# Gate on expert rows at the PSUM exit, hidden activations turned in halves, block sums behind the gathers: one change to a fused attention, expert and dense kernel

## The chip, the cores and the metric

One core of a Trainium2 chip. The metric is the device time of one launch, in microseconds (us). Engines: TensorE (PE; its weight loads are PEld), VectorE (DVE), ScalarE (ACT), GpSimd (POOL), SyncE (SP, which only issues DMAs); an engine's queue takes its instructions in order.

## The reference

```python
state = gamma*state + k[t] outer v[t];  y[t] = scale * q[t] @ state   # 4 batches, 8 heads, 768 steps, 64 wide
x = rows of y                                    # 3072 tokens x 512
logits = x @ w_gate + modality_bias[modality_id] # 8 experts
e = argmax(logits);  gate = softmax(logits)[e]
x = gate * (relu(x @ w1[e]) @ w2[e])             # w1 512x1024, w2 1024x512
h = x @ w_in;  out = (h * sigmoid(1.702*h)) @ w_out   # 2048 wide
```

## The kernel before

**Order of the work.** Attention over 24 tiles of 128 tokens writes x to HBM (x_rows). DVE works out the routing: tokens are sorted by expert into slots, each expert's slots padded to whole tiles of 128. With these inputs three experts get tokens, 13, 12 and 1 tiles, so used_tiles is 26 (the 26 stores of y_slots agree). Then the expert tiles run, and then the dense part in three groups of 1024 tokens: eight pairs of column blocks up (seven products each, P1, P5, P6, P3, P7, P2, P4), and the way down. All products are in three passes (hi*hi, hi*lo, lo*hi: L1519, L1520, L1521); a value's hi part is a copy by ACT, its lo part a subtraction by DVE.

**An expert tile i** (expert_step). PE: up(i), 24 multiplications; turn_rows, which turns the gathered x of tile i+1; down(i-1), 24 multiplications into ps_y, which needs both halves of hT_lo of tile i-1 and all of w2; turn_hidden(i), eight transposes (L1566). ACT: relu of the two halves of up(i) (L809), xT_hi(i+1), hT_hi(i) in two halves, and the issue of the stores of y(i-1). DVE: xT_lo(i+1) (L1146), take_y(i-1) (a copy of the slots' token numbers, L1229, and the copy of ps_y to y_out, L1230), then hT_lo(i) in two halves (L1206). The first 15 tiles are stored twice, to y_head and to y_slots.

**POOL's queue**, in order. gather_slots for tiles 0 to 4 (five buffers xg): a copy of indices (L569) and an indirect DMA (L571). pool_step(0): the gather of tile 5 and, where an expert begins (T_SPLIT), the split of the next expert's weights, eight pieces: a casting DMA (L589) and a subtraction (L578) each. Then two load_quads (L666), two mix_quads (four block sums, L673 to L678, and a store to w_comb, L681), and three rounds of: two load_quads, then five pool_step(k), with a mix_quads behind the second and third. pool_step(k) waits for gT_done of tile k, gathers tile k+5, and may split weights. After tile 15 come fetch_first (rows of y_head for the first group by L625, for each tile of tokens a gather of gates by L632, and the scaling by the gate, L639), more pool_steps, and for the later groups fetch: rows by L625, gates by L632; there ACT scales the rows (scale_rows, L872) behind pairs 2 and 5. At the end POOL scatters the output by indirect DMA (store_half, L688) and waits for out_stored.

**The loop over tiles that may not exist.** ACT and DVE run i from 24 to 30 with a test i < used_tiles, so that empty turns come behind the last tile.

## Time and profile before

| | us |
|---|---|
| median of 3 runs | 1022.33 |
| lowest, highest | 1018.75, 1022.68 |
| the profiled execution, its own time | 1028.59 |
| its span | 1027.0 |
| PE busy in the span | 967.7 |

The span runs from the first record to the last of one profiled execution; that execution has a time of its own beside the three runs. Busy time is the sum of an engine's instructions. The granted clock is a share of full speed.

### The profile page before, as it was taken

Reading aid. Unit: us, or ns where it says so; the run is one execution under the profiler, and the core shown is the slowest. Engines: PE = TensorE matmul, PEld = TensorE weight load, DVE = VectorE, ACT = ScalarE, POOL = GpSimd, SP = SyncE. Lnnn points to the kernel's source line nnn. Section 1 sums busy time; section 2 is a strip of 40 time slices with the busy share of each in tenths; the row PEclk is TensorE's granted clock in tenths of the full one; section 3 lists DMA queues with packets and bytes.
Section 4 is the critical chain, followed back from the end, with each engine's and each line's share of the span. In section 5 each row is a group of like instructions: output and inputs, shape, how many; then the busy total and the mean of one; then the engine's idle time right before and its main releaser. Section 6 shows DMA issues by size and latency. Waiting matters only on the chain.

```text
span 1027.0 us, 16695 instructions
## 1 busy us (share of the span) xinstructions
PE 967.7 (94%) x5947; PEld 786.6 (77%) x5948; DVE 470.5 (46%) x706; ACT 416.3 (41%) x672; POOL 254.1 (25%) x287
## 2 busy tenths in 40 slices
PE   7999789959999989999899999999999999999995
PEld 5778557848888868888678788877788888888884
DVE  2444384212222212214656586446668545665541
ACT  2333323212222212222666664446666445564441
POOL 4444143665124772200033001051200101000101
PEclk8999989979999999999999999999999999999998
DMA  8778357776236542100344124363313535222431
GB/s 277 242 248 240 113 208 261 231 254 216 107 130 223 182 137 72 50 25 25 120 145 125 57 86 144 104 224 106 121 51 94 144 118 183 90 82 83 142 103 42
DMA packets 50968, 143.86 MB, mean 140 GB/s; under 512 B 6092, under 2 KB 6260, under 8 KB 46788
## 3 DMA queue, kind: packets, MB, share of 16 engines
q1 hardware_dynamic: 29904, 84.97, 25.9%
q0 software_dynamic: 11440, 40.74, 11.8%
q10 hardware_dynamic: 9540, 17.10, 4.7%
q8 instruction: 45, 0.74, 0.3%
q14 instruction: 39, 0.32, 0.1%
HBM read 100.81 MB, written 33.59 MB: 131 GB/s over the span
## 4 chain that ended last, share of the span: by engine, by line
PE 83%; DMA 5%; issue 4%; ACT 3%; DVE 3%; POOL 2%; SPq 0%; POOLq 0%; ACTq 0%; DVEq 0%
PE bank L1519 23%; PE bank L1521 23%; PE bank L1520 23%; DMA raw<-w 2%; PE bank L1398 2%; PE bank L1424 2%; PE bank L1566 2%; PE bank L1433 1%; PE bank L1414 1%; PE bank L1385 1%; PE bank L1601 1%; PE bank L1528 1%; POOL weights L578 1%; PE bank L1444 1%; DMA qk_in<-qk 1%
## 5 line engine op out<-in xcount | busy, mean ns | idle before, releaser
L1521 PE MATMUL bank<-w_hi,act_lo 128*128 128x512 f32 x384 | 150.3, 391 | 0.0
L1519 PE MATMUL bank<-w_hi,act_hi 128*128 128x512 f32 x384 | 150.1, 391 | 0.0
L1520 PE MATMUL bank<-comb_lo,act_hi 128*128 128x512 f32 x384 | 150.0, 391 | 0.0
L1519 PE MATMUL bank<-mix_hi,w_hi 128*128 128x512 f32 x336 | 133.7, 398 | 10.0 <-ACT h_sum L738 8.0
L1521 PE MATMUL bank<-mix_hi,comb_lo 128*128 128x512 f32 x336 | 133.0, 396 | 0.0
L1520 PE MATMUL bank<-mix_lo,w_hi 128*128 128x512 f32 x336 | 132.1, 393 | 0.0
L738 ACT ACTIVATE w_hi<-comb 128x1024 fp32r<-128x1024 f32 x96 | 96.0, 1002 | 81.0 <-PE bank L1521 75.6
L688 POOL DMA_INDIRECT out<-f_out,token_idx x24 | 25.6, 1067 | 389.9 <-ACT f_out L738 383.0
L1282 DVE TENSOR_TENSOR comb_lo<-comb,w_hi 128x1024 fp32r<-128x1024 f32 x48 | 58.8, 1224 | 72.6 <-ACT w_hi L738 71.8
L1519 PE MATMUL bank<-weights,hT_hi 128*128 x208 | 85.9, 413 | 5.5 <-issue 4.0
L1288 DVE TENSOR_TENSOR h_sum<-bank,h_sum 128x512 f32<-128x512 f32 x72 | 49.5, 689 | 84.1 <-PE bank L1521 78.6
L1146 DVE TENSOR_TENSOR xT_lo<-bank,xT_hi 128x512 fp32r<-128x512 f32 x27 | 18.7, 692 | 146.8 <-ACT xT_hi L738 144.8
L1519 PE MATMUL bank<-weights,xT_hi 128*128 x208 | 83.1, 400 | 1.6 <-DVE xT_lo L1146 1.6
L1519 PEld LDWEIGHTS bank<-mix_hi,w_hi 128*128 128x128 f32 x336 | 63.7, 190 | 27.0 <-ACT h_sum L738 10.1
L1520 PEld LDWEIGHTS bank<-comb_lo,act_hi 128*128 128x128 f32 x384 | 72.1, 188 | 15.9
L1521 PEld LDWEIGHTS bank<-w_hi,act_lo 128*128 128x128 f32 x384 | 72.1, 188 | 15.7
L1519 PEld LDWEIGHTS bank<-w_hi,act_hi 128*128 128x128 f32 x384 | 72.1, 188 | 15.7
L1520 PE MATMUL bank<-weights,hT_hi 128*128 x208 | 83.0, 399 | 1.0 <-issue 1.0
L1521 PE MATMUL bank<-weights,hT_lo 128*128 x208 | 83.5, 401 | 0.4 <-issue 0.3
L738 ACT ACTIVATE hT_hi<-bank 128x512 fp32r<-128x512 f32 x52 | 28.3, 595 | 132.2 <-PE bank L1566 126.3
L1521 PE MATMUL bank<-weights,xT_lo 128*128 x208 | 81.5, 392 | 0.0
L1520 PE MATMUL bank<-weights,xT_hi 128*128 x208 | 81.3, 391 | 0.0
(178 smaller groups left out, 1636.9 us busy)
## 6 DMA issues: line engine op xcount, KB each, us to landing
comb<-w_comb SPq DMA_DIRECT2D x24, 1024.0 KB
comb<-w_out SPq DMA_DIRECT2D x48, 512.0 KB
qk_in<-qk SPq DMA_DIRECT2D x24, 512.0 KB, 3.7
raw<-w SPq DMA_DIRECT2D x24, 512.0 KB, 5.9
weights<-raw POOLq DMA_DIRECT2D x16, 512.0 KB, 4.6
w_comb<-mix_in POOLq DMA_DIRECT2D x8, 1024.0 KB, 4.2
y_slots<-y_out ACTq DMA_DIRECT2D x26, 256.5 KB
v_in<-v SPq DMA_DIRECT2D x24, 256.0 KB, 4.5
```

What stands on the lines that cost most here:

```text
L578: nc.gpsimd.tensor_tensor(lo, raw[:, i % RAW_BUFS, :], hi.bitcast(F32), ALU.subtract).then_inc(w_ready, 1)
L688: pool.indirect_dma_start(out=out, out_offset=bass.IndirectOffsetOnAxis(ap=token_idx[:, g % 2, j:j + 1], axis=0), in_=f_out[:, j, :], in_o ...
L738: copy = lambda dst, src: nc.scalar.activation(dst, src, ACT.Copy)
L1146: tt(xT_lo[:, :, :], ps_gT, xT_hi[:, :, :].bitcast(F32), ALU.subtract).then_inc(gT_split, 1)
L1282: tt(comb_lo[piece % COMB_BUFS][:, 0:PIECE], comb_f[piece % COMB_BUFS][:, 0:PIECE], w_hi[piece % HI_BUFS][:, 0:PIECE].bitcast(F32), ALU.su ...
L1288: tt(h_sum[:, at_, :], bank[k % 2][:, :], h_sum[:, at_, :], ALU.add).then_inc(h_ready, 1)
L1398: last = mm(ps_scores[par][keys, p, :], kT[rows, t % 2, p, keys], turned[rows, p, :], start=True, stop=True)
L1424: last = mm(x_place(h), v_in[:, t % IN_BUFS, h, :], masked[:, t % 2, (h % 2) * PAIRS + h // 2, :], start=(t % CHUNKS == 0 and h < 4), stop ...
L1519: mm(dst, hi, w_hi, start=first, stop=False, skip_group_check=skip)
L1520: mm(dst, hi, w_lo, start=False, stop=False, skip_group_check=skip)
L1521: return mm(dst, lo, w_hi, start=False, stop=last, skip_group_check=skip)
L1566: last = turn(ps_hT[s][:, a, :], hid[:, s * 4 + a, :], identity)
```

## The change

Gates by slot: POOL gathers the five first tiles' gates right behind gather_slots(0 to 4), and in pool_step(k), k > 0, that of tile k+4, after y_copied has reached k+1. take_y multiplies ps_y by the gate where it copied, and the scaling by POOL and ACT and the gathers of gates by token row are gone. y_copied now starts at 1, by a small copy of DVE ahead of its tile loop, behind which DVE waits for the five first gates. ACT turns gateT and stores gate_rows earlier.

Halves: down(i-1) and turn_hidden(i) are cut in two and alternate. DVE takes y behind hT_lo, and down waits for y_copied. The last tile's down goes into bank 6, and its take_y and store move into the first pair of the first group.

Block sums: the two first mix_quads and the two first load_quads of each round move behind pool_steps. The rest: a Sigmoid of one column behind hidden_hi(0); the empty turns of the tile loop come first on ACT and DVE; a pool.drain() ahead of the last group's stores, and the wait for out_stored moved from POOL to SP.

The core of the diff (declarations, the two fetch functions' calls of keep_index and the empty lines are left out):

```diff
@@ -204,7 +206,8 @@
         token_idx = keep("token_idx", [P, 2, GT], I32)
-        row_gate = keep("row_gate", [P, GT], F32)
+        sig_warm = keep("sig_warm", [P, 1], F32)
+        gate_slot = keep("gate_slot", [P, XG_BUFS], F32)
@@ -512,6 +516,7 @@
                     load_piece(g, k)
+            sp.wait_ge(out_stored, DMA_INC * GT * GROUPS)
@@ -572,6 +577,11 @@
                     xg_in[buf], DMA_INC)
+            def gather_gate(buf, tokens):
+                pool.indirect_dma_start(out=gate_slot[:, buf:buf + 1], out_offset=None, in_=gate_rows,
+                                        in_offset=bass.IndirectOffsetOnAxis(ap=tokens, axis=0)).then_inc(gate_in, DMA_INC)
@@ -591,11 +601,17 @@
                         take_lo(i, place(i), n_cast)
-            def pool_step(k, buf):
+            def pool_step(k, buf, first=False):
...
                     gather_slots(k + XG_BUFS, buf)
+                    if not first:
+                        hold(gate_in, DMA_INC * k + DMA_INC * (XG_BUFS - 1))
+                        hold(y_copied, k + 1)
+                        earlier = (buf - 1) % XG_BUFS
+                        gather_gate(earlier, slot_idx[:, earlier:earlier + 1])
@@ -615,9 +631,12 @@
                 gather_slots(k, k)
+            hold(gate_stored, DMA_INC)
+            for buf in range(XG_BUFS):
+                gather_gate(buf, token_of_slot[:, buf:buf + 1])
...
             used_tiles = steering(pool, T_TILES, TILES, MAX_TILES)
-            pool_step(0, 0)
+            pool_step(0, 0, True)
@@ -626,18 +645,10 @@
                                         ).then_inc(yg_in[j], DMA_INC)
-            def gather_gate(g, j, rows):
-                hold(yg_in[j], DMA_INC * g + DMA_INC)
-                pool.indirect_dma_start(out=row_gate[:, j:j + 1], out_offset=None, in_=gate_rows,
-                                        in_offset=bass.IndirectOffsetOnAxis(ap=rows[:, DM:ROW].bitcast(I32), axis=0)
-                                        ).then_inc(row_gate_in[j], DMA_INC)
+            def keep_index(g, j, rows):
+                pool.wait_ge(yg_in[j], DMA_INC * g + DMA_INC)
                 nc.gpsimd.tensor_copy(token_idx[:, g % 2, j:j + 1], rows[:, DM:ROW].bitcast(I32)).then_inc(token_idx_ready, 1)
-            def scale_first(j, rows):
-                pool.wait_ge(row_gate_in[j], DMA_INC)
-                nc.gpsimd.tensor_tensor(rows[:, 0:DM], rows[:, 0:DM],
-                                        row_gate[:, j:j + 1].to_broadcast([P, DM]), ALU.mult).then_inc(yg_scaled, 1)
@@ -689,20 +698,20 @@
                         in_=f_out[:, j, :], in_offset=None).then_inc(out_stored, DMA_INC)
-            hold(gate_stored, DMA_INC)
...
                 load_quads(buf, buf)
-            for buf in range(MIX_BUFS):
-                mix_quads(buf, buf, 1)
             with pool.Fori(0, HEAD_LOOPS) as it:
-                for buf in range(MIX_BUFS):
-                    hold(quads_stored[buf], DMA_INC * it + DMA_INC)
-                    load_quads(it * MIX_BUFS + (MIX_BUFS + buf), buf)
...
                     if 1 <= j <= MIX_BUFS:
-                        mix_quads(it * MIX_BUFS + (MIX_BUFS + j - 1), j - 1, it + 2)
+                        mix_quads(it * MIX_BUFS + (j - 1), j - 1, it + 1)
+                    if j > MIX_BUFS:
+                        buf = j - MIX_BUFS - 1
+                        hold(quads_stored[buf], DMA_INC * it + DMA_INC)
+                        load_quads(it * MIX_BUFS + (MIX_BUFS + buf), buf)
+            for buf in range(MIX_BUFS):
+                mix_quads(HEAD_LOOPS * MIX_BUFS + buf, buf, HEAD_LOOPS + 1)
@@ -724,13 +733,14 @@
             for g in range(1, GROUPS):
+                if g + 1 == GROUPS:
+                    pool.drain()
...
                 store_half(g, 1)
-            hold(out_stored, DMA_INC * GT * GROUPS)
@@ -797,7 +807,7 @@
             def store_y(k, head=False):
-                act.wait_ge(y_copied, k + 1)
+                act.wait_ge(y_copied, k + 2)
@@ -815,16 +825,16 @@
                     copy(hT_hi[:, s * 4:(s + 1) * 4, :], ps_hT[s]).then_inc(hT_hi_done, 1)
+            act.wait_ge(gateT_done, 1)
+            copy(gateT[:, :], ps_gate).then_inc(gateT_copied, 1)
...
             x_hi(1)
+            act.wait_ge(gateT_copied, 1)
+            act.dma_start(gate_rows.rearrange("(t p) a -> t (p a)", p=P), gateT[:, :]).then_inc(gate_stored, DMA_INC)
...
                 first_hi(i)
-            act.wait_ge(gateT_done, 1)
-            copy(gateT[:, :], ps_gate).then_inc(gateT_copied, 1)
-            act.wait_ge(gateT_copied, 1)
-            act.dma_start(gate_rows.rearrange("(t p) a -> t (p a)", p=P), gateT[:, :]).then_inc(gate_stored, DMA_INC)
             hidden_hi(0)
+            nc.scalar.activation(sig_warm[:, :], c_("identity")[:, 0:1], ACT.Sigmoid)
@@ -857,19 +867,15 @@
                     expert_step(READY_TILE + j // 2, False)
-            with act.Fori(TILES, 1 + TILE_LOOPS * XG_BUFS) as i:
-                with act.If(i < used_tiles):
-                    expert_step(i, False)
+            with act.Fori(TILES, MAX_TILES) as i:
+                with act.If(i + used_tiles >= TILES + MAX_TILES):
+                    before = nc.s_assert_within(act.snap((i + used_tiles + (TILE_CYCLE - MAX_TILES - 1)) % TILE_CYCLE),
+                                                TILES - 1, MAX_TILES - 2)
+                    expert_step(before + 1, False)
...
                 copy(mix_hi[:, product, :, :], src).then_inc(x_hi_done, 1)
-            def scale_rows(g, tiles):
-                for j in tiles:
-                    act.wait_ge(row_gate_in[j], DMA_INC * (g + 1))
-                    rows = yg[:, j % ROW_BUFS, 0:DM]
-                    nc.scalar.activation(rows, rows, ACT.Copy, scale=row_gate[:, j:j + 1]).then_inc(yg_scaled, 1)
@@ -952,7 +958,6 @@
                         split_x(0, P4, xT4[:, 1])
-                        store_y(last_tile)
@@ -965,13 +970,13 @@
                     sigmoid_sum(g, k, 0, k, 1)
+                    if first:
+                        store_y(last_tile)
...
                     sigmoid_sum(g, k, 2, k, 0)
-                    if g + 1 < GROUPS and (k + 1, P3) in TURN_AFTER:
-                        scale_rows(g + 1, TURN_AFTER[k + 1, P3] + TURN_AFTER[k + 1, P7])
@@ -1221,19 +1226,23 @@
             last_rank = steering(dve, last_tile + T_RANK, 0, NE - 1)
-            def take_y(k, head=False):
+            def take_y(k, head=False, bank=ps_y):
...
                 nc.vector.tensor_copy(y_out[:, DM:ROW].bitcast(I32), token_of_slot[:, bass.ds(k, 1)])
-                nc.vector.tensor_copy(y_out[:, 0:DM], ps_y[:, :]).then_inc(y_copied, 1)
+                dve.wait_ge(gate_in, DMA_INC * k + DMA_INC)
+                tt(y_out[:, 0:DM], bank[:, :], gate_slot[:, bass.ds(k % XG_BUFS, 1)].to_broadcast([P, DM]), ALU.mult).then_inc(
+                    y_copied, 1)
...
                 x_lo(i + 1)
+                hidden_lo(i)
                 take_y(i - 1, head)
-                hidden_lo(i)
+            nc.vector.tensor_copy(y_out[:, DM:ROW].bitcast(I32), token_of_slot[:, 0:1]).then_inc(y_copied, 1)
+            dve.wait_ge(gate_in, DMA_INC * XG_BUFS)
@@ -1249,6 +1258,7 @@
             dve.wait_ge(fT_copied, GT)
+            dve.wait_ge(token_idx_ready, GT)
@@ -1256,9 +1266,11 @@
             mix_x(0, xT4[:, 1], xT4[:, 2], first_mix[:, 1])
-            with dve.Fori(TILES, 1 + TILE_LOOPS * XG_BUFS) as i:
-                with dve.If(i < used_tiles):
-                    expert_step(i, False)
+            with dve.Fori(TILES, MAX_TILES) as i:
+                with dve.If(i + used_tiles >= TILES + MAX_TILES):
+                    before = nc.s_assert_within(dve.snap((i + used_tiles + (TILE_CYCLE - MAX_TILES - 1)) % TILE_CYCLE),
+                                                TILES - 1, MAX_TILES - 2)
+                    expert_step(before + 1, False)
@@ -1326,7 +1338,6 @@
                 split_x(0, product, src)
-            take_y(last_tile)
@@ -1342,6 +1353,8 @@
                         out_lo(g, 0)
+                    if g == 0 and k == 0:
+                        take_y(last_tile, bank=ps_last)
@@ -1545,26 +1558,25 @@
                             last.then_inc(hid_done, 1)
-            def down(k, rank, at_slot):
-                pe.wait_ge(w_ready, EXPERT_PIECES * rank + EXPERT_PIECES)
-                for f in range(FEC):
-                    if f % (FEC // HALVES) == 0:
-                        pe.wait_ge(hT_split, HALVES * k + (f // (FEC // HALVES) + 1))
+            def down(k, rank, at_slot, half, bank=ps_y):
+                pe.wait_ge(hT_split, HALVES * k + (half + 1))
+                if half == 0:
+                    pe.wait_ge(w_ready, EXPERT_PIECES * rank + EXPERT_PIECES)
+                    pe.wait_ge(y_copied, k + 1)
+                for f in range(half * FEC // HALVES, (half + 1) * FEC // HALVES):
                     col = f * DM
-                    last = split_products(ps_y[:, :], hT_hi[:, f, :], hT_lo[:, f, :],
+                    last = split_products(bank[:, :], hT_hi[:, f, :], hT_lo[:, f, :],
...
                                           W[:, bass.ds(at_slot + (W2_LO + col), DM)], f == 0, f == FEC - 1)
-                last.then_inc(y_done, 1)
-            def turn_hidden(k):
-                wait(pe, hT_split, HALVES * k)
-                for s in range(HALVES):
-                    pe.wait_ge(hid_copied, HALVES * k + (s + 1))
-                    for a in range(4):
-                        last = turn(ps_hT[s][:, a, :], hid[:, s * 4 + a, :], identity)
-                    last.then_inc(hT_done, 1)
+                if half == HALVES - 1:
+                    last.then_inc(y_done, 1)
+            def turn_hidden(k, s):
+                pe.wait_ge(hid_copied, HALVES * k + (s + 1))
+                for a in range(4):
+                    last = turn(ps_hT[s][:, a, :], hid[:, s * 4 + a, :], identity)
+                last.then_inc(hT_done, 1)
@@ -1573,15 +1585,18 @@
             turn_rows(1, 1, DMA_INC)
-            turn_hidden(0)
+            for s in range(HALVES):
+                turn_hidden(0, s)
...
                 rank = steering(pe, i + (T_RANK - 1), 0, NE - 1)
-                down(i - 1, rank, pe.snap(slot_at(rank, n_used)))
-                turn_hidden(i)
+                at_slot = pe.snap(slot_at(rank, n_used))
+                for s in range(HALVES):
+                    down(i - 1, rank, at_slot, s)
+                    turn_hidden(i, s)
@@ -1595,8 +1610,10 @@
             def turn_tokens(g, j, rows):
-                pe.wait_ge(yg_scaled, GT * g + j + 1)
+                pe.wait_ge(yg_in[j], DMA_INC * g + DMA_INC)
                 wait(pe, fT_copied, GT * g + j - 1)
+                if g == 1 and j == 0:
+                    pe.wait_ge(y_copied, used_tiles + 1)
@@ -1619,7 +1636,10 @@
             rank = steering(pe, last_tile + T_RANK, 0, NE - 1)
-            down(last_tile, rank, pe.snap(slot_at(rank, n_used)))
+            at_slot = pe.snap(slot_at(rank, n_used))
+            pe.wait_ge(fT_copied, GT)
+            for s in range(HALVES):
+                down(last_tile, rank, at_slot, s, ps_last)
```

## Rows read from the trace of the kernel before

**Rows 1.** Busy time by stretch: PE, PEld, DVE, ACT, POOL, granted clock, DMA share, GB/s.

```profile
205.00:235.00 30.00, 19.29 (x84) 15.54 (x83) 4.77 (x9) 3.97 (x7) 18.56 (x30) 0.77 0.68 252
235.00:371.00 136.00, 136.00 (x665) 113.14 (x664) 30.05 (x55) 30.48 (x55) 57.98 (x67) 1.00 0.53 178
371.00:385.00 14.00, 10.55 (x42) 7.78 (x41) 1.21 (x3) 1.60 (x4) 13.11 (x19) 0.88 0.13 39
...
512.00:635.00 123.00, 118.79 (x527) 96.84 (x526) 84.01 (x107) 77.51 (x118) 24.65 (x28) 0.99 0.35 110
```

**Rows 2.** PE's waits: total us, times, longest.

```profile
PE bank L1528 <- DMA gathered<-x_rows,slot_idx: 10.7, 1, 10.7
PE bank L1519 <- ACT h_sum L738: 8.0, 5, 1.9
...
PE bank L1519 <- DVE h_sum L1288: 1.4, 1, 1.4
```

**Rows 3.** Timeline of PE, turn_hidden of tiles 4, 5 and 6: start, us.

```profile
205.02 1.03 PE L1566 MATMUL bank<-consts,hid 128*128 128x128 f32 x8
...
230.86 1.04 PE L1566 MATMUL bank<-consts,hid 128*128 128x128 f32 x8
...
243.12 1.03 PE L1566 MATMUL bank<-consts,hid 128*128 128x128 f32 x8
```

**Rows 4.** The chain that ended last, turn_hidden of tiles 16 and 17.

```profile
366.22 0.87 PE bank L1566 x8
...
384.24 1.14 PE bank L1566 x8
```

**Rows 5.** Timeline of POOL, from the gather of tile 5 to the first block sum.

```profile
152.54 1.63 POOL L571 DMA_INDIRECT gathered<-x_rows,slot_idx  x1 [0.79 <-POOL slot_idx L569]
164.11 0.58 POOL L589 DMA_DIRECT2D weights<-raw  x1 [9.94 <-DMA raw<-w]
...
198.20 1.10 POOL L666 DMA_DIRECT2D mix_in<-w_in  x2
203.75 0.73 POOL L673 TENSOR_TENSOR mix_in<-mix_in 128x256 f32<-128x256 f32 x1 [4.45 <-DMA mix_in<-w_in]
```

**Rows 6.** The chain, the piece ahead of PE's restart.

```profile
217.92 4.28 DMA gathered<-x_rows,slot_idx
```

**Rows 7.** Timelines around down(0): ACT, DVE, PE.

```profile
157.77 0.25 ACT L738 ACTIVATE gateT<-bank 24x128 f32<-24x128 f32 x1
158.05 0.56 ACTq L826 DMA_DIRECT2D gate_rows<-gateT  x1
...
162.60 0.48 PE L1519 MATMUL bank<-weights,hT_hi 128*128 x1
...
162.73 0.18 DVE L1219 CAST slot_of_place<-r_slot 128x24 int32<-128x24 f32 x1
164.91 0.69 DVE L1146 TENSOR_TENSOR xT_lo<-bank,xT_hi 128x512 fp32r<-128x512 f32 x1 [2.00 <-issue]
```

**Rows 8.** DMA issues: gathers of gates, last number median us to landing.

```profile
row_gate<-gate_rows,y_gathered POOLq DMA_INDIRECT x16, 3.0
```

**Rows 9.** Timeline of ACT between pairs 2 and 3 of the first group.

```profile
530.64 2.55 ACT L872 ACTIVATE y_gathered<-y_gathered,row_gate 128x512 f32<-128x512 f32 x4
```

**Rows 10.** Timelines of DVE and ACT around the last tile.

```profile
487.43 1.29 DVE L1206 TENSOR_TENSOR hT_lo<-bank,hT_hi 128x512 fp32r<-128x512 f32 x2
...
506.42 0.68 DVE L1230 COPY y_out<-bank 128x512 f32<-128x512 f32 x1
...
508.75 1.28 ACT L900 ACT_TABLE_LOAD   x1
```

**Rows 11.** Timeline: POOL's last store.

```profile
1016.29 0.96 POOL L688 DMA_INDIRECT out<-f_out,token_idx  x1 [0.52 <-issue]
```

**Rows 12.** The records of the closing line, POOL's own: count, ns min/median/max, start.

```profile
L175 POOLq DRAIN  x1: 7753/7753/7753, 1019.1 to 1019.1; - x1
```

**Rows 13.** The records of the program's first line.

```profile
L1728 POOLq DRAIN  x1: 184/184/184, 0.6 to 0.6; - x1
```

More of the change, by code:

```diff
@@ L52 @@
 HEAD_TILES = GT + NE - 1
+TILE_CYCLE = 32
+assert TILE_CYCLE > MAX_TILES and MAX_TILES == 1 + TILE_LOOPS * XG_BUFS
 READY_LOOPS = (TILES - 1) // XG_BUFS
@@ L340, in build @@
         ps_gT, ps_hid, ps_hT, ps_y = quad(0), [banks[1], banks[2]], [quad(3), quad(4)], banks[5]
+        ps_last = banks[6]
         ps_fT, ps_out = [quad(6), quad(7)], banks[0:HT]
@@ L380, in build @@
         yg_in = [sem(f"yg_in{j}") for j in range(GT)]
-        row_gate_in = [sem(f"row_gate_in{j}") for j in range(GT)]
-        yg_scaled, fT_done, fT_copied = sem("yg_scaled"), sem("fT_done"), sem("fT_copied")
+        gate_in = sem("gate_in")
+        fT_done, fT_copied = sem("fT_done"), sem("fT_copied")
         x_mixed, x_hi_done, x_split = sem("x_mixed"), sem("x_hi_done"), sem("x_split")
@@ L649, in fetch_first @@
                 for j in tiles:
-                    gather_gate(0, j, rows[j])
-                for j in tiles:
-                    scale_first(j, rows[j])
+                    keep_index(0, j, rows[j])
             def fetch(g, tiles):
@@ L661, in fetch @@
                 for j in tiles:
-                    gather_gate(g, j, rows[j])
+                    keep_index(g, j, rows[j])
             def load_quads(r, buf):
@@ L866, in split_x @@
                 copy(mix_hi[:, product, :, :], src).then_inc(x_hi_done, 1)
-            def scale_rows(g, tiles):
-                for j in tiles:
-                    act.wait_ge(row_gate_in[j], DMA_INC * (g + 1))
-                    rows = yg[:, j % ROW_BUFS, 0:DM]
-                    nc.scalar.activation(rows, rows, ACT.Copy, scale=row_gate[:, j:j + 1]).then_inc(yg_scaled, 1)
             def early_hi(g, k):
```

## The prediction

> **What bounds the kernel now.** I read busy time by stretch first. PE is the bound: between 235 and 371 us it is busy 136.00 of 136.00 us, and where it isn't, time is lost. It idles 10.7 us between 205 and 235, 3.5 between 371 and 385, and 4.2 between 512 and 635 [rows 1]. So the question of each edit is whether it touches one of PE's gaps. PE's waits name them: 10.7 us in one wait for the gathered rows of an expert tile, 8.0 us in five waits for ACT's copies in the dense part (four of 1.9 and one of 0.4), 1.4 us for DVE's sums [rows 2]. Per tile PE needs 243.12 - 230.86 = 12.26 us, and the turn with the big wait took 230.86 - 205.02 = 25.84, which is 13.6 more: the wait and, behind it, a lower granted clock, 0.77 on average over that stretch [rows 1, 3].
>
> One gap has no cause that I can find. Tile 17 took 384.24 - 366.22 = 18.02 us, 5.8 over the usual [rows 4]; PE, ACT and DVE all stood and only POOL went on. The profiled execution took 1028.59 us, 6.3 over the median of the three runs, so I take it that this gap is the profiled execution's own: 1028.59 - 5.8 = 1022.8, the median within 0.5. The sum below therefore makes no use of it and is applied to 1022.3.
>
> **Block sums behind the gathers.** POOL ends the first split of weights at 198.20 us; then come two loads of w_in, whose landing is awaited until 203.75, both block sums, their stores, two more loads that wait for these, and only then the gather of tile 6, at 217.92, which lands 4.28 us later [rows 5, 6]. PE wanted it at about 211.5. With the change the gather stands behind two load issues. But POOL gets more work ahead of the split: it waits for the stored gates (the store is issued at 158.05, two to three us earlier in the new order, so about 158.5 with its landing) and issues five gathers of gates at some 1.3 us (0.96 for an indirect DMA and its issue gap [rows 11]), to 164.9; the gather of tile 5, at 152.54 before, follows, and the first casting DMA goes from 164.11 to about 168 [rows 5, 7]. Four us later for the whole split, since each further piece waits for a raw buffer that the piece before it frees: end at 202, loads issued to 203.3, gather of tile 6 at about 204.5, landed 4.3 to 5.5 us later (it may queue behind the w_in loads), 209 to 210. PE asks for it at 211.5 plus what it is held up before, 2.3 us (below), 213.8. So the wait goes, with 4 us to spare: **-13.6**. If it came 3 us late PE would lose 3 us and a part of the clock, so I bound the term by -9 and -13.6. Later block sums have slack: weights for the third expert are needed only at the 26th tile, the quads only at the first dense group.
>
> **The first y_copied.** down(0) now waits for a copy which DVE makes behind the place computation and three register loads. down(0) began at 162.60; the last cast of that computation is at 162.73 and DVE's next instruction came only at 164.91, 2.0 us of issue ahead of it [rows 7]. The new copy takes that place. ACT reaches hidden_hi(0) about 0.5 earlier, as 0.25 of gateT and 0.56 of its store left from ahead of it, so y_copied comes at 164.6; but gateT's 0.25 now delays the first relu, on which PE waits. I count **+2.3** in all, 1.5 to 2.8. DVE next waits for the five gates: last issued at 164.9, landing 3.0 later [rows 8], 167.9, then xT_lo(2) at 0.7, needed by PE at about 171. That is covered, but by 2.5 us only; a landing after 5.5 us, as that of the w_in loads [rows 5], would cost up to 1 more.
>
> **Halves.** As many transposes and multiplications as before; two more changes between the kinds per tile. I take 0.02 us a tile, **+0.5** over 25; bounds 0 and 0.1 a tile, 2.5. The new wait: take_y(i-1) stands behind hT_lo(i), so y_copied comes about 2.4 us after the last transpose (0.64 for a copy of 512 columns by ACT [rows 9], 0.64 of DVE for the second half, 0.15 and 0.68 for y [rows 10], and the hand-overs). A tile's 12.26 us less 12 transposes (0.87 for eight [rows 4], so 1.3) are 0.228 us for each of 48 multiplications; down(i) follows the 24 of up(i+1), 5.5 us, and four transposes, 0.4: slack 3.5 us. Nor does the earlier turn of the first half wait: relu is done 1.3 us after up, and 2.7 us of down lie between. Steady tiles win nothing either, for PE had no gap there [rows 1].
> The product with the gate instead of the copy reads the same 512 columns from PSUM as L1206 does, 0.69 against 0.68. Gates of later tiles are asked for five tiles ahead, one indirect DMA of 1 us per 12.3 us of POOL. POOL is now held to the end of tile k in pool_step(k); behind it stand only the gather of tile k+6 (needed four tiles later) and the split for an expert that starts twelve tiles later.
>
> **No scaling by ACT.** Ahead of pair 3 ACT scales four tiles of rows, 2.55 us, just before the copies that PE waits for [rows 9]; the same stands ahead of pair 6 and twice in the second group. Four waits of 1.9 go: 8.0 less the odd one of 0.4 [rows 2], **-7.6**. ACT's next work was late by 1.9 of 2.55, so it then has 0.6 in hand; if the sums by DVE are next in the way, one half stays: bounds -4 and -7.6. POOL also loses 24 gathers of gates and eight scalings, hidden before (it waited for PE) and hidden now.
>
> **Around the last tile.** DVE's copy of y, 0.84 with the tokens', leaves the chain to P4's sum on which PE waits 1.4 [rows 2, 10]: -0.7. ACT's table load of 1.28 [rows 10] goes to a place where ACT waited 2.0 for PE, and the empty turns go ahead of the last tiles: -0.6 from the small waits behind it. Against that down(25) waits for take_y(24), which now follows the last hT_lo (487.43 and 1.29) by 0.8, where it needed only the first half: +0.5. Net **-0.8**, bounds -2 and +0.5.
> By the Trainium skill, "ScalarE: Activation LUTs", section "Table sets: the hidden batching unit", Relu and Copy are in every set, so that the early Sigmoid costs one load and no later ones. The trace shows Copy beside Sigmoid under one load, and no Relu under that set. If Relu were not there, two loads a tile would still lie in ACT's idle time.
>
> **The end.** The last store is issued to 1017.25, POOL waits for its landing, and then a drain of POOL takes 7.75 us, 1019.1 to 1026.9, the last thing in the span; the same instruction took 0.18 at the start, with no DMA before it [rows 11 to 13]. With SP waiting for the landing, POOL's drain begins at 1017.3, so at least 1.8 goes if it costs 7.75 again, unless it is a wait for DMA that can't start sooner (0). If it is work that piled up over the 133 DMAs POOL issued, the drain put ahead of the last group pays it under 100 us of PE's work, and 8 stores are left: the end is then at about 1019.4, -7.6. The two rows, none and all, speak for work that piles up. I take **-6.0**.
> The Trainium skill, "VectorE: DVE Perf Modes", section "The DRAIN you can't avoid", calls the drains of the runtime's frame about 12 ns on all engines. The 7.75 us here disagree; by that rule this term would be nil.
>
> **Sum.** -13.6 +2.3 +0.5 -7.6 -0.8 -6.0 = -25.2, from 1022.3: **997 us**.
>
> **Rivals.**
> A. The gather of tile 6 is still late (its landing queues behind w_in, or the gates' gathers take twice as long in the busy stretch). For it: the DMA share of 0.68 there [rows 1]. Against: 4 us to spare. Price 4 to 6: 1002.
> B. The last drain costs what it did. Price 4.2 to 6: 1002.
> C. The wait for a gather only moves to a later tile (0 for -13.6), DVE's sums take half of ACT's place (-4) and the drain costs what it did (-1.8): with the rest -3.8, 1018.5, no change. Against: behind tile 6 POOL needs under 10 us for each 12.3 us of PE.
> D. Slower: the chain hT_lo, take_y, y_copied, down outruns up(i+1) at each tile. It decides when y_copied comes 6.9 us after the last transpose instead of 2.4: 3.5 of slack, and 1.0 more at each of 25 tiles to eat up the 25 gained. At 1.3 us a tile beyond the slack, as when each tile's gate lands late: +32.5 -25.2, 1030. Against: gates are asked for five tiles ahead.
> E. The odd gap of tile 17 is in the timed runs too, and goes with the gathers of gates that POOL issued while all stood: 991.
>
> **How the numbers follow.** As forecast 0.50, A 0.12, B 0.18, E 0.10, C 0.06, D 0.04. The range of the forecast's own terms is 993 to 1002; with A and B together, and E, 988 to 1007. A change under 0.5%, 5.1 us, I take as none: faster 0.90, same 0.06, slower 0.04.
>
> **What would show it.** In the profile after: no wait for gathered rows, and a granted clock near 1.00 between 205 and 235; a PE gap of about 2 us before down(0); 12.3 us per tile; no 1.9 us waits for ACT in the dense part; POOL's closing drain under 1 us, and a second one in the last group. Wrong: a wait of PE on y_copied per tile, table loads within the tile loop, or a closing drain of 7 us.

## The result and the profile after

| | before | after |
|---|---|---|
| median of four runs, us | 1020.98 | 987.96 |
| lowest to highest, us | 1018.75 to 1022.68 | 985.12 to 991.18 |
| profiled execution: time, span | 1028.59, 1027.0 | 991.18, 989.6 |

The ratio is 0.9679 (0.9641 to 0.9717): 33 us less. Run again later (a_again) it was 0.9619 (0.9579 to 0.9659). 997.0 had been forecast, with 988 to 1007 as the range: the median lies 9 us under the number and at the range's very end. The range of the forecast's own terms, 993 to 1002, was missed.

The two profiled executions are 37.4 us apart, more than the medians, because that of before was an unusually long one. Busy time by stretch of the kernel after answers to [rows 1]; the first row is the stretch of down(0), and the last two lie in the dense part:

```profile
157.00:175.00 18.00, 14.69 (x63) 11.88 (x63) 8.76 (x17) 6.86 (x11) 11.59 (x13) 0.91 0.63 222
205.00:235.00 30.00, 30.00 (x149) 24.80 (x148) 6.85 (x12) 7.31 (x13) 14.91 (x21) 1.00 0.66 229
371.00:385.00 14.00, 14.00 (x72) 11.57 (x71) 3.08 (x6) 3.48 (x6) 11.33 (x15) 1.00 0.67 254
505.00:630.00 125.00, 125.00 (x565) 103.08 (x564) 84.44 (x107) 73.02 (x109) 11.98 (x16) 1.00 0.36 114
690.00:830.00 140.00, 140.00 (x622) 115.21 (x621) 88.89 (x111) 76.02 (x111) 13.79 (x16) 1.00 0.37 121
```

Between 205 and 235 us, where PE had been busy for 19.29 of 30, it is busy throughout at a granted clock of 1.00. The dense stretches have no gap either. A new gap of 2.4 us stands in the first row; the rest of the 3.3 us idle there, 0.9, is a wait for xT_lo that the kernel before has as well. PE's waits say what is left, and answer to [rows 2]:

```profile
PE bank L1437 <- issue: 4.8, 1, 4.8
...
PE bank L1532 <- DVE y_out L1244: 2.4, 1, 2.4
PE bank L1532 <- DVE y_out L1236: 2.2, 1, 2.2
...
PE bank L1532 <- ACT h_sum L748: 0.8, 1, 0.8
...
PE bank L1532 <- DVE h_sum L1300: 0.7, 1, 0.7
```

The 10.7 us for gathered rows and the waits of 1.9 for ACT are gone. Two waits for y_out are new: L1244 is the first y_copied, and L1236 is tile 24's y, for which the last down waits. The 4.8 at L1437 lie in the attention, which the change doesn't touch (3.2 in the kernel before, at L1424).

POOL's timeline answers to [rows 5]:

```profile
168.49 1.80 POOL L599 DMA_DIRECT2D weights<-raw  x3 [0.84 <-issue]
...
198.35 1.10 POOL L675 DMA_DIRECT2D mix_in<-w_in  x2
200.45 1.02 POOL L576 DMA_INDIRECT gathered<-x_rows,slot_idx  x1 [0.80 <-POOL slot_idx L574]
...
212.38 0.75 POOL L682 TENSOR_TENSOR mix_in<-mix_in 128x256 f32<-128x256 f32 x1
```

The gather of tile 6 is issued at 200.45 instead of 217.92 [rows 6], and the block sum comes after it. The split began four us later than before but ended at the same 198 us.

**Where the 37.4 us went.** Both kernels do the same 5947 PE instructions in nearly the same order. Setting the start of each beside that of its counterpart gives how far the kernel after is ahead at each; the steps of that lead, read at the same place within a tile, are the account. It is worked out from the two traces, to about 0.1 us a row, and is no view of either.

| place | lead gained, us | the prediction's term |
|---|---|---|
| up to down(0) (attention, tile 0) | -1.3 | none |
| down(0): first y_copied | -4.3 | -2.3 |
| gather of tile 6 | +13.5 | +13.6 |
| tile 17 and the one behind it | +6.0 | left out, as the profiled execution's own |
| all other tiles (halves) | -0.3 | -0.5 |
| around the last tile | +3.7 | +0.8 |
| dense part, ACT's scaling | +12.6 | +7.6 |
| from PE's last multiplication to the end | +7.5 | +6.0 |

### The profile page after: what moved, and what is told of

It is laid out like the page before. It is cut to its first block, busy times and chain, and to the rows that moved or that the text cites. A ratio compares the mean times of both kernels' runs of the same rounds, so it can differ in the third digit from the quotient of the medians.

```text
span 989.6 us, 16790 instructions
## 1 busy us (share of the span) xinstructions
PE 959.0 (97%) x5947; PEld 781.7 (79%) x5948; DVE 469.8 (47%) x707; ACT 410.6 (41%) x657; POOL 245.6 (25%) x281
## 4 chain that ended last, share of the span: by engine, by line
PE 93%; DVE 3%; issue 2%; ACT 1%; DMA 1%; DVEq 0%; POOL 0%; SPq 0%; POOLq 0%; ACTq 0%
PE bank L1532 26%; PE bank L1534 26%; PE bank L1533 26%; PE bank L1437 2%; PE bank L1411 2%; PE bank L1578 2%; PE bank L1398 1%; PE bank L1427 1%; PE bank L1446 1%; PE bank L1541 1%; PE bank L1618 1%; PE bank L1457 1%; DMA qk_in<-qk 1%; PE bank L1465 1%; PE bank L1389 1%
## 5 line engine op out<-in xcount | busy, mean ns | idle before, releaser
L748 ACT ACTIVATE w_hi<-comb 128x1024 fp32r<-128x1024 f32 x96 | 96.0, 1002 | 77.5 <-PE bank L1534 75.1
L1211 DVE TENSOR_TENSOR hT_lo<-bank,hT_hi 128x512 fp32r<-128x512 f32 x52 | 35.9, 691 | 120.7 <-ACT hT_hi L748 120.7
L748 ACT ACTIVATE hT_hi<-bank 128x512 fp32r<-128x512 f32 x52 | 31.0, 599 | 132.7 <-PE bank L1578 132.7
```

Source lines behind the costliest of these rows:

```text
L748: copy = lambda dst, src: nc.scalar.activation(dst, src, ACT.Copy)
L1211: tt(hT_lo[:, part, :], ps_hT[s], hT_hi[:, part, :].bitcast(F32), ALU.subtract).then_inc(hT_split, 1)
```

## The experiments

Twelve kernels ran, in three groups, each group beside runs of the kernel before on the same chip (medians of before: 1025.5, 1027.8 and 1019.9 us). Ratios are to before on that chip. "b" kernels are the kernel before with one part of the change, "a" kernels the kernel after with one part undone or altered.

**b_sums.** The kernel before, with nothing but the new order of block sums and loads (the hunk of the change at pool's round loop):

```diff
-            for buf in range(MIX_BUFS):
-                mix_quads(buf, buf, 1)
             with pool.Fori(0, HEAD_LOOPS) as it:
-                for buf in range(MIX_BUFS):
-                    hold(quads_stored[buf], DMA_INC * it + DMA_INC)
-                    load_quads(it * MIX_BUFS + (MIX_BUFS + buf), buf)
...
```

> The kernel before with one part of the change alone: the two first mix_quads and each round's load_quads stand behind the pool_steps. Theory (the gather of tile 6 waited behind the block sums, and a lowered clock followed the wait): PE's wait of 10.7 us for the gathered rows goes, tile 5 takes 12.3 us instead of 25.8, and the time falls by 13 to 14 us, to about 1007. Rival (the wait only moves to a later gather, because POOL's queue is as full as before): PE waits for gathered rows elsewhere and the time falls by less than 5 us. Rival on the clock (the slower multiplications behind the wait are not its consequence): the wait goes, the time falls by 10.7 and not more.

Measured: 1010.79 us, ratio 0.9845 (0.9783 to 0.9907), 10 to 22 us less. The windows of that kernel show the stretch of tile 5:

```profile
198.00:228.00 30.00, 30.00 (x147) 24.94 (x146) 6.16 (x11) 7.22 (x13) 16.77 (x26) 1.00 0.86 290
```

PE has no gap and the full clock, and tile 5 takes 12.3 us instead of 25.8. The timed runs alone would leave room for 10.7 us, the wait without the low clock behind it; the tile's time doesn't. The term is shown, and no other part of the change is needed for it.

**b_drain.** The kernel before, with POOL's drain ahead of the last group's stores and the wait for the output's landing on SP:

```diff
+            sp.wait_ge(out_stored, DMA_INC * GT * GROUPS)
...
+                if g + 1 == GROUPS:
+                    pool.drain()
...
-            hold(out_stored, DMA_INC * GT * GROUPS)
```

> The kernel before with only the end changed: a pool.drain() ahead of the last group's stores, and the wait for the landed output on SP instead of POOL. Theory (POOL's closing drain is work that piles up over its DMAs): the closing drain falls from 7.75 us to 1 to 4 us, the span's end comes 7 to 7.5 us earlier, time 1013 to 1014. Rival (a fixed cost, only started earlier): the drain stays near 7.75 us and the time falls by 1.8 us, to about 1019.

Measured: 1019.69 us, ratio 0.9964 (0.9940 to 0.9989). Its records of the two drains, the new one and the closing one, are

```profile
L729 POOLq DRAIN  x1: 9737/9737/9737, 846.1 to 846.1; - x1
...
L175 POOLq DRAIN  x1: 3257/3257/3257, 1010.5 to 1010.5; - x1
```

In the profile the way from PE's last multiplication (ends 1009.2) to the end of the span (1014.0) is 4.8 us; it was 12.3 before. So 7.5 us go in the profile, while the timed runs give 1.1 to 6.1 (the medians are 5.8 apart). The difference between them isn't explained.

A record's length is not what the drain adds. The closing one begins 0.2 us ahead of the last store's own record (1010.72, 0.96 long) and ends 2.1 behind it, 0.1 after SP has passed its wait for the landing. So what the eight stores behind the early drain leave to pay can't be told from the wait for the landing.

**b_noscale.** The kernel before, but ACT leaves the rows of the second and third group as they are: the gates are left out of their sum.

```diff
                     act.wait_ge(row_gate_in[j], DMA_INC * (g + 1))
-                    rows = yg[:, j % ROW_BUFS, 0:DM]
-                    nc.scalar.activation(rows, rows, ACT.Copy, scale=row_gate[:, j:j + 1]).then_inc(yg_scaled, 1)
+                    act.sem_inc(yg_scaled, 1)
```

> The kernel before, in which ACT does not scale the gathered rows of the second and third group (their gates are left out of the output; their gathers stay). Theory (the four waits of 1.9 us and, behind the second of each group, a stretch at the lower granted clock both come from the 2.55 us of scaling): the waits go, the granted clock stays up in the dense part, and the time falls by 11.5 to 12.5 us, to about 1009. Rival (the prediction's sum, waits alone): the time falls by 7.6 us and a lowered clock stays near 570 and 745 us.

Measured: 1012.53 us, ratio 0.9874 (0.9825 to 0.9923), 8 to 18 us less (7.9 at the least): more than the 7.6 of the four waits. Two windows of the kernel before, behind the second wait of each group, say why:

```profile
567.00:575.00 8.00, 7.30 (x32) 6.00 (x33) 2.12 (x4) 4.27 (x8) 0.00 (x0) 0.79 0.00 0
...
741.00:749.00 8.00, 6.57 (x26) 5.37 (x27) 2.34 (x3) 4.90 (x9) 0.00 (x0) 0.79 0.00 1
```

and one of b_noscale over the first group:

```profile
512.00:635.00 123.00, 123.00 (x556) 101.41 (x555) 85.94 (x109) 73.70 (x110) 22.51 (x26) 1.00 0.37 114
```

At 0.79 on average, PE ran part of each short window at the lower level of 1.2 GHz: each multiplication from 569.0 to 571.9 takes 0.43 us from start to start and those on either side 0.23. By the alignment that costs 1.6 us behind each of the two second waits, and each of the four waits itself about 2.1. Without the scaling neither the waits nor the low clock are there.

How often the clock falls differs from execution to execution. Five profiles have these four waits of 1.9: the clock fell behind two of them in that of before, behind three in those of b_sums, b_nofirstscale and b_nofirstgate, and behind one in that of b_drain. First b_sums at the first wait, then b_drain at the fourth:

```profile
510.00:520.00 10.00, 8.11 (x31) 6.24 (x30) 5.19 (x7) 7.18 (x12) 0.00 (x0) 0.87 0.30 107
```
```profile
737.00:745.00 8.00, 6.55 (x37) 5.62 (x38) 3.50 (x5) 5.82 (x11) 0.00 (x0) 1.00 0.01 3
```

By these, an estimate of the scaling's price is 10 to 13 us (four times 2.1, and one to three times 1.6).

**a_nodrain.** The kernel after without its pool.drain():

```diff
-                if g + 1 == GROUPS:
-                    pool.drain()
```

> The changed kernel without the drain ahead of the last group; SP still waits for the output. Theory (work that piles up): the closing drain is 7 to 9 us again and starts at the last store's end, so the time is 4 to 5.5 us over that of the changed kernel, about 993. Rival (moving the wait to SP was what helped): the closing drain stays near the 3.3 us of the changed kernel and the time at 988.

Measured: 994.44 us, ratio 0.9711 (0.9666 to 0.9757). The closing drain:

```profile
L177 POOLq DRAIN  x1: 7147/7147/7147, 987.9 to 987.9; - x1
```

From PE's last multiplication (ends 986.6) to the end of the span (995.3) it is 8.7 us. With b_drain this divides the term: 12.3 to 8.7 by SP waiting in POOL's place, 8.7 to 4.8 by the early drain. The division is the profiles'; the kernel after did not run beside it, and the two ratios, 0.9711 and 0.9679, have overlapping intervals.

**a_again.** The kernel after, unchanged, on another chip, as the base of the next three.

> The changed kernel once more, as the measure for the three beside it: all theories expect 0.968 of the kernel before.

Measured: 989.1 us, ratio 0.9619 (0.9579 to 0.9659).

**a_oldsums.** The kernel after with the old order of sums and loads (the edit of b_sums, reversed).

> The changed kernel with the block sums and the w_in loads where the kernel before has them. Theory: POOL ends its weight split at about 198 us as before, so the gather of tile 6 is issued near 218 us again and lands near 222.5; PE, now 5.5 us later in its tiles, asks for it at 217, waits 5 to 6 us and then runs about 2 us behind at the lower granted clock: 7 to 8 us over the changed kernel. Rival (the order of the sums gives the full 13.6 us here too): 13 us over it. Rival (the gates of all tiles now cost POOL so much that the sums no longer decide): under 2 us over it.

Measured: 999.17 us, ratio 0.9734 (0.9690 to 0.9777), 10 us over a_again, more than the 7 to 8 expected. Its wait of PE and its gather:

```profile
PE bank L1540 <- DMA gathered<-x_rows,slot_idx: 8.2, 1, 8.2
```
```profile
215.81 1.02 POOL L576 DMA_INDIRECT gathered<-x_rows,slot_idx  x1 [0.80 <-POOL slot_idx L574]
```

With the old order alone the wait is back where it was. It is 2.5 us shorter than before because the gather is issued at 215.81 instead of 217.92 and lands in 4.0 us instead of 4.3, while PE comes to it at the same 211.5: everything up to down(0) happened to be earlier in this execution (162.50, against 166.53 in the kernel after), which made up for the wait on the first y_copied. And behind that wait, 2.4 us long here too, the clock stayed up: the window 157 to 175 has 1.00.

**a_whole.** The kernel after with both halves of down ahead of both halves of the turn:

```diff
                     down(i - 1, rank, at_slot, s)
+                for s in range(HALVES):
                     turn_hidden(i, s)
```

> The changed kernel with the halves undone: both halves of down, then both of turn_hidden. Theory (steady tiles have no gap that the halves could fill, and alternating costs nothing): tiles stay at 12.3 us; only the last down, which waits for the last take_y, starts 0.6 to 1 us later; time the same within 0.2%. Rival (alternating costs PE time at every change between transposes and multiplications): 1 to 2.5 us less. Rival (the halves keep y_copied off the path): with them undone each tile's down waits, over 12.4 us a tile, and the time is more than 3 us over.

Measured: 987.09 us, ratio 0.9613 (0.9570 to 0.9656). In the timed runs the halves change nothing that can be measured. Its profile has every steady tile at 12.29 us, that of a_again 12.30 and 12.32 in turn. The last down still waits 2.4 us for y_out.

**a_best.** The kernel after, with the first y_copied counted behind hidden_lo(0) instead of behind the places, and no wait on y_copied for the last down, which writes a bank of its own:

```diff
             hidden_lo(0)
+            nc.vector.tensor_copy(y_out[:, DM:ROW].bitcast(I32), token_of_slot[:, 0:1]).then_inc(y_copied, 1)
...
-            nc.vector.tensor_copy(y_out[:, DM:ROW].bitcast(I32), token_of_slot[:, 0:1]).then_inc(y_copied, 1)
...
-                    pe.wait_ge(y_copied, k + 1)
+                    if bank is ps_y:
+                        pe.wait_ge(y_copied, k + 1)
```

> The changed kernel, with the first count of y_copied made right behind hT_lo(0) instead of behind the place computation and register loads, and without the wait of the last tile's down for y_copied, which a bank of its own doesn't need. Theory: the wait of 2.4 us at down(0) and the lower granted clock behind it go (2.4 and 1.7 us), and of the 2.2 us at the last down about 1 goes; time 4 to 5 us under the changed kernel, about 0.963 of the kernel before. Rival (PE would then wait for the five gates, through DVE's next subtraction, which the late copy hid): a new wait of 1 to 3 us ahead of tile 2's products, and under 2 us are won.

Measured: 985.23 us, ratio 0.9575 (0.9534 to 0.9616), about 4 us under a_again; the two intervals overlap. The window of down(0):

```profile
157.00:175.00 18.00, 18.00 (x81) 14.70 (x81) 7.98 (x18) 5.82 (x10) 12.69 (x13) 0.93 0.72 242
```

PE is busy for 18.00 of 18.00 us where it was for 14.69 after the change, and both waits for y_out are gone from its list. The clock in that window, 0.93, is hardly above the 0.91 of the kernel after, but the low stretch is another one: it runs from 156.2 to 159.6, ahead of down(0) at 163.7, behind two short waits of 1.1 and 0.9 that end at 156.1. From down(0) on each multiplication takes 0.23 us.

**b_nofirstscale and b_nofirstgate.** The kernel before. In the first, POOL doesn't scale the first group's rows; in the second it doesn't gather their gates either. Both leave the gates out of that group's sum.

```diff
                 for j in tiles:
-                    scale_first(j, rows[j])
+                    pool.wait_ge(row_gate_in[j], DMA_INC)
+                    pool.sem_inc(yg_scaled, 1)
...
```

This is the first's edit. The second replaces the gathers of gates by the copy of the token numbers alone.

> The kernel before, in which POOL does not scale the rows of the first group (their gate is left out of the output; all gathers stay). For the slow tile 17 (18.3 us in the profile before, 15.6 to 17.3 in two of its variants, 12.3 in every profile of the changed kernel). Theory 1 (the gathers of gates slow all engines' queues down): the slow tile stays. Theory 2 (POOL's multiplications do, through something DVE or PE share with POOL): it is gone, 12.3 us. Theory 3 (neither: the new loop body that ACT and DVE enter there): it stays here and in the kernel beside this.

> The kernel before, in which POOL neither gathers the gates of the first group nor scales its rows (their gate is left out of the output). Theory 1 (gathers of gates): no slow tile, time 3 to 6 us under the kernel before. Theory 2 (multiplications): no slow tile either, and none in the kernel beside this. Theory 3 (a new loop body): tile 17 takes 15 us or more still.

Measured: 1020.01 us, 1.0008 (0.9983 to 1.0034), and 1018.76 us, 1.0010 (0.9981 to 1.0040). The windows over tile 17, first of the kernel before, then of these two:

```profile
366.00:385.00 19.00, 15.55 (x68) 12.01 (x66) 3.25 (x7) 2.68 (x6) 16.91 (x23) 0.91 0.31 87
```
```profile
366.00:385.00 19.00, 19.00 (x95) 15.85 (x94) 4.65 (x9) 5.13 (x10) 12.99 (x22) 1.00 0.43 118
```
```profile
366.00:385.00 19.00, 19.00 (x93) 15.77 (x92) 3.42 (x6) 4.46 (x8) 7.75 (x17) 1.00 0.44 121
```

The slow tile is in neither profile. Yet neither kernel is faster, and their intervals leave room for 1.7 and 1.9 us of gain, not for 6.0. So either the timed runs of before mostly don't have the slow tile, or something as large is lost elsewhere.

**a_best_whole and a_oldloop.** a_best with the halves undone as in a_whole; and the kernel after with the old tile loops on ACT and DVE, whose empty turns come last:

```diff
-            with dve.Fori(TILES, MAX_TILES) as i:
-                with dve.If(i + used_tiles >= TILES + MAX_TILES):
...
+            with dve.Fori(TILES, 1 + TILE_LOOPS * XG_BUFS) as i:
+                with dve.If(i < used_tiles):
+                    expert_step(i, False)
```

> The two edits of the better version (early first count of y_copied, no wait of the last down for it) with the halves undone. Theory (halves are worth nothing): the same time as with the halves within 0.2%, about 0.957 of the kernel before. Rival (the halves shorten the last tile's chain once its wait is gone): 1 us more.

> The changed kernel with the loops of ACT and DVE over the last tiles in their old form, empty turns last. Theory (PE's gap of 2.0 us in the last down and the lower clock behind it came from PE's own code, not from ACT and DVE): that gap stays away; ACT and DVE begin the dense part 2 us later, which PE's last down covers; time within 1 us of the changed kernel. Rival (the gap of 2 us was a wait for what ACT and DVE do late): it comes back, 3 to 4 us over the changed kernel.

Measured: 986.16 us, 0.9664 (0.9628 to 0.9699), and 990.14 us, 0.9715 (0.9683 to 0.9746). Neither a_best nor the kernel after ran on this chip, and ratios don't carry over: the medians of before differ by 8 us between this chip and a_best's, those of a_oldloop and a_again by 1. So a_best_whole misses the expected 0.957 and lies 1 us from a_best. What stands on one chip is that a_best_whole is 4.0 us under a_oldloop, as a_best is 3.9 under a_again; so the halves bring nothing in a_best that can be seen. In a_oldloop the 2.0 us stop of PE inside the last down, discussed below, didn't come back, so it doesn't hang on the loops of ACT and DVE.

## Why the prediction was right, and where it was off

**As a whole.** Three parts, each made alone, give -1.55%, -1.26% and -0.36%: together -3.17%, against -3.21% (the result) and -3.81% (a_again) for the whole change (each is known to some 0.3 to 0.6%, so the closeness to the first is chance in part). The block sums and the scaling are most of it. By the profiles, without tile 17, the gain is 37.4 - 6.0 = 31.4 us where 25.2 had been forecast. The 6.2 between are +5.0 for the scaling, +2.9 around the last tile, +1.5 at the end, +0.2 for the halves, less 2.0 at the first y_copied, 1.3 ahead of it and 0.1 at tile 6.

The mechanisms of the large terms were right, but that a median of 988 was still in the range is luck in part. The range reached below 993 for rival E, a tile 17 that is slow in the timed runs too. That isn't shown, and what filled the place is, for the larger part, lower clocks and a stop of PE that the sum did not hold.

**Block sums behind the gathers (-13.6): right**, by b_sums, a_oldsums and the alignment. One step of its working was wrong and harmless: the split was to end at 202 us, four later. It began four later and ended at 198.35, so the pieces had had that much slack in their waits for raw buffers. Rivals A and C, a gather late there or later, are out: PE's list has no wait for gathered rows.

**No scaling by ACT (-7.6): the mechanism was right, the term too small**; 12.6 by the alignment of these two profiles. What failed is "four waits of 1.9 go", taken as the whole price. For the wait of tile 6 the prediction did count the lower clock behind it; for these it did not, though its own row had a clock of 0.99 over that stretch [rows 1]. The four waits at 2.1 are 8.4, the low clock behind the two second ones 3.2, and a small wait near 684 us 0.65: 12.3 of the 12.6. Another execution of before would have given some 1.6 less or more, as the clock fell behind one to three of the waits.

**The first y_copied (+2.3): the same omission.** PE's wait was 2.4, as worked out:

```profile
164.03 0.40 DVE L1224 CAST slot_of_place<-r_slot 128x24 int32<-128x24 f32 x1
...
166.05 0.15 DVE L1244 COPY y_out<-token_of_slot 128x1 int32<-128x1 int32 x1 [1.62 <-issue]
169.22 0.69 DVE L1151 TENSOR_TENSOR xT_lo<-bank,xT_hi 128x512 fp32r<-128x512 f32 x1 [3.01 <-DMA gate_slot<-gate_rows,token_of_slot]
```

DVE's 1.62 us of issue ahead of a copy of 0.15 are most of what PE waits for. The wait puts down(0) 2.6 us back against the kernel before. And behind it PE runs at the lower level from 167.3 to 170.7, which is another 1.7: 4.3 in all. Of the six profiles with this wait five have that low stretch; a_oldsums has not. Then DVE waits 3.0 for the gates, and PE doesn't wait for DVE there, as foreseen. a_best removes the wait.

**Halves (+0.5): +0.3.** Tiles take 12.29 and 12.33 us in turn against 12.29, under 0.02 a tile as forecast, and too little for the timed runs. Rival D, the chain over y_copied at each tile, needed a wait in every tile; there is none.

**Around the last tile (-0.8): -3.7, and the larger part was not foreseen.** The last down waits 2.2 where it waited 1.4, and PE's wait for DVE's sum fell from 1.4 to 0.7; both had been counted. Not counted was a stop of PE in the middle of the last down, of which the kernel before has two rows:

```profile
491.25 0.39 PE L1521 MATMUL bank<-weights,hT_lo 128*128 x1
493.67 0.63 PE L1519 MATMUL bank<-weights,hT_hi 128*128 x1 [2.03 <-issue]
```

It is between the halves of the product, whose second needs hT_lo's second half; DVE had that done at 488.7. It is followed by 3.4 us at the lower clock (each multiplication 0.43 from start to start), another 1.7. Both are gone after the change. PE's waits of the kernel before held four such "issue" waits at L1519:

```profile
PE bank L1519 <- issue: 4.3, 4, 2.0
```

Two of them are tile 17's; no step used the longest. a_oldloop shows that the new loops of ACT and DVE are not what removed it, so it hangs on PE's own new code, or on where that code lies.

The packets of the DMA queue that the profile calls "instruction" (q8, 16384 bytes each) point to a wait for code. In the kernel before one of them runs from 491.3 to 492.2, and PE goes on 1.5 us behind it. All six profiles with the old PE code have this stop behind the twelfth of 24 multiplications, 1.7 to 2.6 us long, and in all PE goes on 1.5 to 1.6 us behind such a packet. So it does, 1.1 to 1.5 us behind one, after the long issue wait in the attention in all 14 profiles. In the kernel after that packet runs from 474.2 to 475.6, while PE waits for y_out anyway. In a_best_whole, without that wait, a stop of 1.0 us stands three multiplications further on in the same down, again 1.4 behind a packet. It is a coincidence found many times, and no run tests it. The clock fell behind the stop in two of the six profiles (before and b_drain), so 1.7 of the 3.7 belong to this execution.

The early Sigmoid did what was said: ACT's only table load in this part is now

```profile
159.88 1.28 ACT L837 ACT_TABLE_LOAD   x1
```

and it lies in a stretch where ACT had to wait for PE anyway. The Trainium skill, "ScalarE: Activation LUTs", section "Table sets: the hidden batching unit", has Relu and Copy in every set. The trace agrees: behind this one load ACT does 25 tiles of Relu and Copy, and then the Sigmoids, with no other.

**The end (-6.0): 7.5 in the profile, 1.1 to 6.1 in the timed runs of b_drain.** The records of after, answering to [rows 12]:

```profile
L737 POOLq DRAIN  x1: 8710/8710/8710, 821.7 to 821.7; - x1
...
L177 POOLq DRAIN  x1: 3259/3259/3259, 986.1 to 986.1; - x1
...
L177 SPq DRAIN  x1: 7/7/7, 989.2 to 989.2; - x1
```

The reading that the drain is work which piles up holds: 8.7 us are paid at 821.7, under PE's work, and the closing one falls from 7.1 without it to 3.3. That it is POOL's DMAs which pile it up, and not its other instructions, isn't separated. The step "closing drain under 1 us" is wrong for the record, which takes 3.3; but 1.2 of these lie under the last store and the rest under the landing, as in b_drain. It is the landing that limits the end now as well: SP comes past its wait at 989.2, and POOL's drain ends at 989.4. The 7.5 are the whole of what the prediction gave to a drain with nothing left to pay (7.6), of which it took 6.0. Rival B, a last drain of the old price, is out.
The Trainium skill, "VectorE: DVE Perf Modes", section "The DRAIN you can't avoid", gives about 12 ns to the drains of the runtime's frame. SP's of 7 ns here agrees; POOL's of 3259 and 7147 ns do not.

**Tile 17 (rival E): open.** The profile of before lost 5.7 us there and 0.3 in the tile behind. It was taken as belonging to that execution alone, and two kernels whose profile lacks it are not faster. But it is not a single accident: b_drain's profile has that tile at 16.8 us and b_noscale's at 15.6, b_sums' loses 1.8 in the next two, and none of the kernels without the first group's gates has it, nor any with the change. The stop begins at 375.4, while POOL still gathers gates and before its multiplications at 378.78, so these are not what starts it. Nor are the gathers alone: b_nofirstscale keeps them and has no slow tile. Whether the timed runs share it would need their traces.

## What to carry to other kernels

Price a wait of PE by its length and by what the granted clock may do behind it: a low stretch behind a wait of 1.9 or 2.4 us cost another 1.6 to 1.7 here. It came behind 12 of 20 waits of 1.9 and 5 of 6 of 2.4 at down(0), so it belongs into the range as well as the sum. This forecast left it out of two of its terms, in opposite directions. A gather that another engine needs next goes ahead, in its queue, of block sums that are needed much later. When a semaphore starts at a higher count, put its first signal where the engine has already passed by, not behind the next block of address work.

## What the runs showed of the hardware

- POOL's drain took 0.18 us before any DMA, 7.15 to 7.75 at the end of a kernel with no drain between, 8.7 and 9.7 at five sixths of it (1.3 of these under the store ahead), and 3.3 at the end when a drain had stood ahead of the last group. It is no wait for the output's landing alone: in the kernel before it began after the landing.
- PE's clock fell to 1.2 GHz behind waits of 2.4 us at down(0) in five profiles of six. Behind the four waits of 1.9 in the dense part it fell in three of five profiles at the first, in all at the second, in none at the third and in four at the fourth. The same wait can have either outcome.
- PE stopped for 1.7 to 2.6 us with no wait that the profile shows, in the middle of the last down, in all six profiles with the old PE code, and went on 1.5 to 1.6 us behind a packet of the instruction queue. The stops at 375.4 us of the kernel before have no such packet within 10 us, and their cause wasn't found.
